# Attention and two expert layers on one core: the first loads on two queues, masks first, and GpSimd's first rounding moved behind two normalisations

## The chip, the cores and the metric

The program runs on one core of one Trainium2 chip, in one launch. The metric is the device time of that core in microseconds (us). The kernel before takes 1297.48 us, the median of three runs that lie between 1297.32 and 1298.49 us.

A core has five engines that run their own instruction lists and wait for one another by semaphores: TensorE (PE in the profile, with its weight loads as PEld), VectorE (DVE), ScalarE (ACT), GpSimd (POOL) and SyncE (SP). DMA transfers are begun by an instruction on one of them; in the kernel before all are begun by SyncE.

## The reference, cut to what matters

```
x  = attention(q, k, v)      # 2 x 8 heads, 768 positions, 64 wide; keys kept:
                             # the first 4 positions (sinks) and a window of 128
h  = x @ w_in                # 1536 x 512 by 512 x 1024
ln = layernorm(h * softmax(h)) * g_ln
y  = ln @ w_out              # 1536 x 1024 by 1024 x 512
P  = exp(y @ w_gate - max), 8 rounds of dividing by row and by column sums
out = sum over 8 experts e:  P[:, e] * (relu(y @ w1[e]) @ w2[e])
```

Everything is float32. For attention the scores of a query tile are taken with a band of keys and the sinks, a mask is added, and the row is exponentiated, divided by its sum and multiplied by the values.

## The kernel before, in words

The attention stage goes over 8 pairs of heads (p = 0 to 7); the two heads of a pair (h = 0, 1) lie in the lower and the upper 64 partitions of `q_sb` and `k_sb`. A pair has six tiles of 128 queries (t = 0 to 5). For each tile PE makes the scores (L659), DVE adds the mask and takes the row maximum (`mask_max`, L1202), ACT exponentiates (L982), and after two tiles, a batch b, DVE takes the inverse sums (L1210, L1214). Then the probabilities are scaled: DVE does one block (L1217), ACT one (L997), and POOL the two blocks of head 1 (`normalise`, L493). PE turns them (L679), ACT and DVE copy them out (L989, L1223), PE multiplies by the values (L705) and by the sinks' values (L711), and ACT and DVE write the result in two parts into `xw` (L1001, L1233). The work of one pair overlaps with the next: in PE's order `scores(p + 1, 0)` stands between tile 5 of pair p and `pv(p, 0)`, and `turn_sinks(p)` and `turn(p, 2)` stand inside pair p + 1.

All orders are written out by hand, one list for each engine. Four places matter here.

SyncE begins the loads of q and k of pairs 0 and 1 (`load_qk`, four DMAs for each head, 16 in all), waits until the constants are made, then begins the v loads of pair 0, the first segments of `w_in` and `w_out` (256 KB each, into `w_raw`), the small tables `g_col` and `wg_raw`, and the v loads of pair 1. After that, for p from 1 on, it waits until GpSimd has finished with segment p - 1 (`in_done`, `out_done`) and begins segment p; the q and k loads of pair 2 stand behind segment 1 in the list, and so on.

GpSimd fills four constants (L458 to L461), makes `ident` (L463), and then the three masks (L465 to L485). After that it rounds the first segments of the weights (`round_segments(0)`: L500 and L503, each of which waits for its DMA), and goes round the pairs: normalise batch 0, rest of `w_in` (L509), normalise batch 1, rest of `w_out` (L515), normalise batch 2, rounding of the next segments.

PE waits for all five constants and for all eight q and k loads of pair 0 before its first scores. `turn(p, 0)` needs GpSimd's `normalise(p, 0)`, and `scores(1, 0)` the eight loads of pair 1.

At the end of pair 0 ACT copies the gate weights (L1025), for which it waits for `small_loaded`, and DVE, before `mask_max` of pair 1, waits for that copy and subtracts (L1262).

The stages behind attention (h = x @ w_in, the layer norm, y, the gate, 8 experts in 4 units each) are one stream of matmuls on PE.

Of the kernel before, what the change touches and what calls it, by code (L numbers as in the profile page):

```python
# [24 lines left out]
F32 = mybir.dt.float32  # L25
F32R = mybir.dt.float32r
BF16 = mybir.dt.bfloat16
ALU = mybir.AluOpType
# [32 lines left out]
def solu_moe(nc: bass.Bass, n_sink, window, qT, kT, v, w_in, w_out, g_ln, w_gate, w_exp, out):  # L61
# [5 lines left out]
    with ExitStack() as ctx:  # L67
# [143 lines left out]


        qk_loaded = [sem(f"qk_loaded{h}") for h in range(2)]
        v_loaded = [sem(f"v_loaded{h}") for h in range(2)]
# [150 lines left out]


        @block.sync
        def _(sp):
# [18 lines left out]
            def load_segments(j):  # L387

                sp.dma_start(w_raw[:, 0:BANK], w_in[j]).then_inc(win_loaded, 16)
                sp.dma_start(w_raw[:, BANK:2 * BANK], w_out[j]).then_inc(wout_loaded, 16)  # L390

            for h in range(2):
                load_qk(0, h)
            for h in range(2):
                load_qk(1, h)
            sp.wait_ge(consts, 4)
            for h in range(2):
                load_v(0, h)
            load_segments(0)
# [56 lines left out]
        def _(pool):  # L456

            pool.memset(ident[:, :], 0.0).then_inc(consts, 1)  # L458
            pool.memset(ones[:, :], 1.0).then_inc(consts, 1)
            pool.memset(v_sink[:, :], 0.0).then_inc(consts, 1)  # L460
            pool.memset(wg[:, :, :].bitcast(F32), 0.0).then_inc(consts, 1)  # L461
            pool.wait_ge(consts, 4)
            pool.affine_select(out=ident[:, :], in_=ident[:, :], compare_op=ALU.not_equal, fill=1.0,  # L463
                               base=0, pattern=[[-1, P]], channel_multiplier=1).then_inc(consts, 1)
            pool.memset(mask0[:, :], 0.0)  # L465
            pool.memset(mask1[:, :], 0.0)
            pool.memset(mask2[:, :], 0.0).then_inc(masks, 1)
            pool.wait_ge(masks, 1)

# [14 lines left out]
            pool.memset(mask0[:, 0:NS], 0.0)  # L484
            pool.memset(mask1[:, 0:NS], 0.0).then_inc(masks, 1)  # L485

            def normalise(p, b):
# [29 lines left out]

            round_segments(0)
            for p in range(PAIRS):
                normalise(p, 0)  # L520
                rest_w_in(p)
                normalise(p, 1)
                rest_w_out(p)
                normalise(p, 2)
                if p + 1 < PAIRS:
                    round_segments(p + 1)
# [120 lines left out]
        def _(pe):  # L647
            def scores(p, t):

                if t == 0:  # L650
                    pe.wait_ge(qk_loaded[p % 2], 128 * (p // 2 + 1))
                for h in range(2):
                    k = 2 * t + h
                    n = STEPS * p + k
                    if n >= S_BANKS:
                        pe.wait_ge(scores_read, n - S_BANKS + 1)
                    rows_h = slice(64 * h, 64 * h + 64)
                    w, at = width(t), k_from(t, h)
                    pe.matmul(bank(k % S_BANKS)[:, 0:w], q_sb[rows_h, p % 2, t * P:(t + 1) * P],  # L659
                              k_sb[rows_h, p % 2, k_at(t), at:at + w], start=True, stop=True).then_inc(scores_full, 1)  # L660
# [76 lines left out]
            def h1_half(T, n):  # L737
# [15 lines left out]
                if n == 1:  # L753
                    last.then_inc(h1_full, 1)

            pe.wait_ge(consts, 5)
            scores(0, 0)
            for p in range(PAIRS):
# [218 lines left out]
        @block.scalar  # L977
        def _(act):
            def exp_tile(p, k):
                act.wait_ge(scores_read, STEPS * p + (k + 1))  # L980
# [35 lines left out]
            for p in range(PAIRS):  # L1016
# [6 lines left out]
                if p == 0:  # L1023
                    act.wait_ge(small_loaded, 32)
                    act.activation(wg[:, :, WG_AT:WG_AT + EXPERTS], wg_raw[:, :, :], ACT.Copy).then_inc(wg_ready, 1)  # L1025

# [496 lines left out]
```

## Time and profile before

| | |
|---|---|
| median of three runs | 1297.48 us (1297.32 to 1298.49) |
| the profiled execution | 1299.42 us, its span 1297.6 us |
| PE busy | 1254.1 us (97%) |
| PE weight loads | 1099.6 us (85%) |
| DVE / ACT / POOL busy | 593.6 / 442.1 / 709.5 us |
| mean granted clock of TensorE | 0.996 of full speed |

The span runs from the first to the last instruction. Attention takes the first 110 us of it, some 12.6 us for a pair from pair 2 on; from there to the end PE is busy nearly without a break. The profile gives the granted clock of TensorE as a share of full speed, where 1.00 is 2.4 GHz and 0.50 is 1.2 GHz. "SPq" rows are DMAs being begun by SyncE: the time in them is that of the issue, not of the transfer.

### The profile page before, as it was taken

To read this page: it belongs to the slowest core of one execution; us is meant where nothing else is said; L and a number is where in the kernel's file an instruction comes from. 1 tells how busy PE (TensorE), PEld (TensorE's weight loads), DVE (VectorE), ACT (ScalarE), POOL (GpSimd) and SP (SyncE) were. 2 spreads that over 40 slices of the span, in tenths; PEclk is the share of its full clock that TensorE was granted. 3 is DMA by queue.
4 is the path that set the end of the run, shared out by engine and by line. 5 is a ranking of instruction groups with operands and counts; after the bars stand their busy time and mean duration, and the time that the engine had idled before them with its cause. 6 is when DMAs were issued, how large, how long until landed. Compare 5 with 4: busy or idle time off the path is not lost.

```text
span 1297.6 us, 18947 instructions
## 1 busy us (share of the span) xinstructions
PE 1254.1 (97%) x6462; PEld 1099.6 (85%) x6462; DVE 593.6 (46%) x1155; ACT 442.1 (34%) x1015; POOL 709.5 (55%) x768
## 2 busy tenths in 40 slices
PE   6889999999999999999999999999999999999998
PEld 3556899998888888888888888888888888888887
DVE  4885645334554444444444444444444444444444
ACT  4774534332225222222222222222222222223222
POOL 4553313575555555555555555555555555555652
PEclk8999999999999999999999999999999999999999
DMA  6651000001111111111111111111111111111102
GB/s 156 162 146 46 1 1 1 17 34 33 33 33 33 33 33 33 33 32 32 32 32 32 32 33 32 34 35 35 38 36 33 32 32 32 32 32 33 34 17 97
DMA packets 62607, 53.17 MB, mean 41 GB/s; under 512 B 9824, under 2 KB 49760, under 8 KB 62560
## 3 DMA queue, kind: packets, MB, share of 16 engines
q1 hardware_dynamic: 62560, 52.57, 14.0%
q8 instruction: 27, 0.44, 0.1%
q14 instruction: 20, 0.16, 0.0%
HBM read 49.40 MB, written 3.15 MB: 40 GB/s over the span
## 4 chain that ended last, share of the span: by engine, by line
PE 71%; POOL 14%; issue 10%; DVE 2%; ACT 1%; SPq 1%; POOLq 0%; DMA 0%; DVEq 0%
PE ps L733 23%; PE ps L735 22%; PE ps L734 22%; POOL ring L612 6%; POOL ring L604 5%; POOL ring L600 2%; PE ps L705 1%; PE ps L679 1%; PE ps L783 1%; PE ps L659 1%; DVE pT L1223 1%; PE ps L711 1%; POOL probs L493 1%; ACT probs L982 1%; PE ps L920 1%
## 5 line engine op out<-in xcount | busy, mean ns | idle before, releaser
L612 POOL TENSOR_TENSOR ring<-sums,ring 128x384 fp32r<-128x384 f32 x192 | 194.9, 1016 | 413.7 <-ACT sums L1144 413.7
L1456 DVE SCALAR_TENSOR_TENSOR acc<-ps,gate_now,acc 128x512 f32<-128x512 f32 x336 | 252.3, 751 | 224.8 <-PE ps L735 224.8
L733 PE MATMUL ps<-ring 128*128 128x512 f32 x768 | 303.5, 395 | 17.2 <-POOL ring L612 13.9
L734 PE MATMUL ps<-ring 128*128 128x512 f32 x768 | 299.6, 390 | 0.0
L735 PE MATMUL ps<-ring 128*128 128x512 f32 x768 | 299.4, 390 | 0.0
L1129 ACT ACTIVATE sums<-ps 128x384 f32<-128x384 f32 x192 | 94.4, 492 | 541.2 <-PE ps L735 541.2
L1432 DVE TENSOR_TENSOR sums<-ps,sums 128x384 f32<-128x384 f32 x192 | 106.8, 556 | 259.2 <-ACT sums L1129 162.3
L733 PEld LDWEIGHTS ps<-ring 128*128 128x128 f32 x768 | 144.1, 188 | 54.7 <-issue 27.2
L735 PEld LDWEIGHTS ps<-ring 128*128 128x128 f32 x768 | 144.2, 188 | 30.8
L734 PEld LDWEIGHTS ps<-ring 128*128 128x128 f32 x768 | 144.2, 188 | 25.9
L733 PE MATMUL ps<-xw,ring 128*128 128x384 f32 x448 | 152.4, 340 | 0.5 <-ACT sums L1129 0.4
L735 PE MATMUL ps<-xw,ring 128*128 128x384 f32 x448 | 151.0, 337 | 0.0
L734 PE MATMUL ps<-xw,ring 128*128 128x384 f32 x448 | 150.9, 337 | 0.0
L733 PE MATMUL ps<-xw,w_b 128*128 128x384 f32 x448 | 150.5, 336 | 0.0
L735 PE MATMUL ps<-xw,w_b 128*128 128x384 f32 x448 | 150.3, 336 | 0.0
L734 PE MATMUL ps<-xw,w_b 128*128 128x384 f32 x448 | 150.0, 335 | 0.0
L1143 ACT ACTIVATE ring<-sums 128x384 fp32r<-128x384 f32 x192 | 100.4, 523 | 118.5 <-DVE sums L1432 118.4
L1144 ACT ACTIVATE sums<-sums 128x384 f32<-128x384 f32 x192 | 98.1, 511 | 0.0
L733 PEld LDWEIGHTS ps<-xw,ring 128*128 128x128 f32 x448 | 84.1, 188 | 2.9 <-ACT sums L1129 0.7
L734 PEld LDWEIGHTS ps<-xw,w_b 128*128 128x128 f32 x448 | 84.3, 188 | 2.0
L733 PEld LDWEIGHTS ps<-xw,w_b 128*128 128x128 f32 x448 | 84.1, 188 | 1.8
L734 PEld LDWEIGHTS ps<-xw,ring 128*128 128x128 f32 x448 | 84.1, 188 | 1.8
(141 smaller groups left out, 1728.1 us busy)
## 6 DMA issues: line engine op xcount, KB each, us to landing
w_in<-w_exp SPq DMA_DIRECT2D x64, 256.0 KB, 3.3
w_raw<-w_exp SPq DMA_DIRECT2D x64, 128.0 KB, 2.7
w_raw<-w_exp SPq DMA_DIRECT2D x32, 256.0 KB, 3.1
q_sb<-qT SPq DMA_DIRECT2D x16, 192.0 KB, 3.8
k_sb<-kT SPq DMA_DIRECT2D x16, 192.0 KB, 3.9
v_sb<-v SPq DMA_DIRECT2D x16, 192.0 KB
out<-acc SPq DMA_DIRECT2D x12, 256.0 KB, 2.0
k_sb<-kT SPq DMA_DIRECT2D x16, 128.0 KB, 3.6
```

The costliest lines, as they stand in the source:

```text
L493: last = pool.tensor_tensor(a, a, a_stat[:, A_INV, k:k + 1].to_broadcast([P, width(t)]), ALU.mult)
L600: pool.tensor_scalar(w2c(0, 0, 2 * BANK), w2_raw(0, 2 * BANK), 1.0, 0.0, ALU.mult, ALU.add).then_inc(w2_hi, 1)
L604: last = pool.tensor_tensor(w2c(1, i * BANK, BANK), w2_raw(i * BANK, BANK), w2c(0, i * BANK, BANK).bitcast(F32), ALU.subtract)
L612: pool.tensor_tensor(h_at(1, i, b * BLK, BLK), c_sum(m), h_at(0, i, b * BLK, BLK).bitcast(F32), ALU.subtract).then_inc(h_lo_pool, 1)
L733: pe.matmul(o, ws[0], xs[0], start=first, stop=False, skip_group_check=True)
L734: pe.matmul(o, ws[0], xs[1], start=False, stop=False, skip_group_check=True)
L735: return pe.matmul(o, ws[1], xs[0], start=False, stop=last, skip_group_check=True)
L1129: act.activation(part_sum(m, s), a_bank(s), ACT.Copy).then_inc(part_copied, 1)
L1143: act.activation(h_at(0, i, b * BLK, BLK), c_sum(m), ACT.Relu)
L1144: act.activation(c_sum(m), c_sum(m), ACT.Relu).then_inc(h_hi_out, 1)
L1432: dve.tensor_tensor(c_sum(m), at, part_sum(part, s), ALU.add).then_inc(c_summed, 1)
L1456: dve.scalar_tensor_tensor(out=acc[:, T, :], in0=y_bank(u, T), scalar=gate_now[:, T:T + 1], in1=acc[:, T, :], op0=ALU.mult, op1=ALU.add).t ...
```

## The change

The first pair's q and k loads are begun by two engines, SyncE for head 0 and ScalarE for head 1, with six DMAs each in place of four: the first 256 columns of q and k come first and count on a semaphore of their own, `qk_first`. PE starts its first scores when these have landed, without waiting for the constants; tile 1 waits for the constants, tile 2 for the rest of the pair's loads. SyncE's list goes on with the v loads of pair 0 (for which it waits on two constants, no longer four), and only then with q and k of pair 1. GpSimd makes the masks first and the last three constants behind them. In pair 0 it normalises batches 0 and 1 before it rounds the first segments of the weights. ScalarE waits for the five constants before it copies the gate weights.

```diff
+        def load_first_qk(queue, h):
+            rows_h = slice(64 * h, 64 * h + 64)
+            q_h, k_h = qT[0, h][0:DH], kT[0, h][0:DH]
+            n, at = 2 * P, h * NS
+            queue.dma_start(q_sb[rows_h, 0, 0:n], q_h[:, 0:n]).then_inc(qk_first, 16)
+            queue.dma_start(k_sb[rows_h, 0, 0, at:at + n], k_h[:, 0:n]).then_inc(qk_first, 16)
+            queue.dma_start(k_sb[rows_h, 0, QT // 2:QT - 1, at:at + n],
+                            k_h[:, P:SEQ - P].rearrange("d (a n) -> d a n", n=n)).then_inc(qk_loaded[0], 16)
+            queue.dma_start(q_sb[rows_h, 0, n:SEQ], q_h[:, n:SEQ]).then_inc(qk_loaded[0], 16)
+            queue.dma_start(k_sb[rows_h, 0, 1:QT // 2, at:at + n],
+                            k_h[:, n:SEQ].rearrange("d (a n) -> d a n", n=n)).then_inc(qk_loaded[0], 16)
+            at = (1 - h) * n
+            queue.dma_start(k_sb[rows_h, 0, :, at:at + NS],
+                            k_h[:, 0:NS].unsqueeze(1).to_broadcast([DH, QT - 1, NS])).then_inc(qk_loaded[0], 16)
...
+            load_first_qk(sp, 0)
+            sp.wait_ge(consts, 2)
             for h in range(2):
-                load_qk(0, h)
+                load_v(0, h)
             for h in range(2):
                 load_qk(1, h)
-            sp.wait_ge(consts, 4)
-            for h in range(2):
-                load_v(0, h)
             load_segments(0)
...
-            pool.memset(ident[:, :], 0.0).then_inc(consts, 1)
-            pool.memset(ones[:, :], 1.0).then_inc(consts, 1)
-            pool.memset(v_sink[:, :], 0.0).then_inc(consts, 1)
-            pool.memset(wg[:, :, :].bitcast(F32), 0.0).then_inc(consts, 1)
-            pool.wait_ge(consts, 4)
-            pool.affine_select(out=ident[:, :], ...).then_inc(consts, 1)
             pool.memset(mask0[:, :], 0.0)
             pool.memset(mask1[:, :], 0.0)
             pool.memset(mask2[:, :], 0.0).then_inc(masks, 1)
+            pool.memset(ident[:, :], 0.0).then_inc(consts, 1)
+            pool.memset(v_sink[:, :], 0.0).then_inc(consts, 1)
...
+            pool.wait_ge(consts, 2)
+            pool.affine_select(out=ident[:, :], ...).then_inc(consts, 1)
+            pool.memset(ones[:, :], 1.0).then_inc(consts, 1)
+            pool.memset(wg[:, :, :].bitcast(F32), 0.0).then_inc(consts, 1)
...
-            round_segments(0)
             for p in range(PAIRS):
                 normalise(p, 0)
-                rest_w_in(p)
+                if p > 0:
+                    rest_w_in(p)
                 normalise(p, 1)
+                if p == 0:
+                    round_segments(0)
+                    rest_w_in(0)
                 rest_w_out(p)
...
-                if t == 0:
+                if t == 0 and p == 0:
+                    pe.wait_ge(qk_first, 64)
+                if (p, t) == (0, 2) or p > 0 and t == 0:
                     pe.wait_ge(qk_loaded[p % 2], 128 * (p // 2 + 1))
...
-            pe.wait_ge(consts, 5)
             scores(0, 0)
+            pe.wait_ge(consts, 5)
...
         def _(act):
+            load_first_qk(act, 1)
...
                     act.wait_ge(small_loaded, 32)
+                    act.wait_ge(consts, 5)
```

Where the instructions now stand is shown in three places. First GpSimd, behind the masks and up to the end of pair 0's batch 1, before:

```order
22 L485 MEMSET mask1 128x4
23 L500 TENSOR_SCALAR xw<-w_raw 128x512 [waits win_loaded]
24 L503 TENSOR_SCALAR w_end<-w_raw 128x512 [waits wout_loaded]
25 L493 TENSOR_TENSOR probs<-probs,a_stat 128x128 [waits norm_link]
26 L493 TENSOR_TENSOR probs<-probs,a_stat 128x256
27 L509 TENSOR_TENSOR xw<-w_raw,xw 128x512 [waits in_hi]
28 L493 TENSOR_TENSOR probs<-probs,a_stat 128x260 [waits norm_link]
29 L493 TENSOR_TENSOR probs<-probs,a_stat 128x260
30 L515 TENSOR_TENSOR w_end<-w_raw,w_end 128x512 [waits out_hi]
```

and GpSimd at the same place with the change:

```order
22 L501 MEMSET wg 128x896
23 L509 TENSOR_TENSOR probs<-probs,a_stat 128x128 [waits norm_link]
24 L509 TENSOR_TENSOR probs<-probs,a_stat 128x256
25 L509 TENSOR_TENSOR probs<-probs,a_stat 128x260 [waits norm_link]
26 L509 TENSOR_TENSOR probs<-probs,a_stat 128x260
27 L516 TENSOR_SCALAR xw<-w_raw 128x512 [waits win_loaded]
28 L519 TENSOR_SCALAR w_end<-w_raw 128x512 [waits wout_loaded]
29 L525 TENSOR_TENSOR xw<-w_raw,xw 128x512 [waits in_hi]
30 L531 TENSOR_TENSOR w_end<-w_raw,w_end 128x512 [waits out_hi]
```

The four scalings of probabilities stand ahead of everything that waits for `w_raw`.

Second SyncE, from its last load for pair 0 to the first segment of the weights, before (the rows from 9 on are pair 1's):

```order
8 L379 DMA k_sb<-kT 64x5x4
9 L372 DMA q_sb<-qT 64x768
16 L379 DMA k_sb<-kT 64x5x4
17 L383 DMA v_sb<-v 128x384 [waits consts]
20 L384 DMA v_sink<-v 4x64
21 L389 DMA w_raw<-w_in 128x512
24 L401 DMA wg_raw<-w_gate 128x32
```

and with the change, where rows 7 to 10 are v of pair 0 and rows 11 to 18 are q and k of pair 1:

```order
1 L373 DMA q_sb<-qT 64x256
6 L381 DMA k_sb<-kT 64x5x4
7 L400 DMA v_sb<-v 128x384 [waits consts]
10 L401 DMA v_sink<-v 4x64
11 L389 DMA q_sb<-qT 64x768
18 L396 DMA k_sb<-kT 64x5x4
19 L406 DMA w_raw<-w_in 128x512
22 L417 DMA wg_raw<-w_gate 128x32
```

The last load of pair 1 moves from place 16 to place 18 of the list, the first segment of `w_in` from 21 to 19.

Third PE, its first scores, before:

```order
1 L659 MATMUL ps<-k_sb,q_sb 128x128 [waits qk_loaded0,consts]
2 L659 MATMUL ps<-k_sb,q_sb 128x128
3 L659 MATMUL ps<-k_sb,q_sb 128x256 x2
4 L659 MATMUL ps<-k_sb,q_sb 128x260 [waits scores_read] x8
5 L679 MATMUL ps<-ident,probs 128x128 [waits probs_scaled,probs_ready0]
```

and with the change:

```order
1 L680 MATMUL ps<-k_sb,q_sb 128x128 [waits qk_first]
2 L680 MATMUL ps<-k_sb,q_sb 128x128
3 L680 MATMUL ps<-k_sb,q_sb 128x256 [waits consts]
4 L680 MATMUL ps<-k_sb,q_sb 128x256
5 L680 MATMUL ps<-k_sb,q_sb 128x260 [waits scores_read,qk_loaded0]
6 L680 MATMUL ps<-k_sb,q_sb 128x260 [waits scores_read] x7
7 L700 MATMUL ps<-ident,probs 128x128 [waits probs_scaled,probs_ready0]
```

One wait at the start has become three, one before each of the first three tiles.

## Rows read from the trace of the kernel before

**Rows 1.** Timeline of PE: start us, us, engine line op, operands [idle before].
```profile
8.69 6.09 PE L659 MATMUL ps<-k_sb,q_sb 64*128 64x128 f32 x24 [8.69 <-DMA k_sb<-kT]
14.71 0.55 PE L679 MATMUL ps<-ident,probs 128*128 128x128 f32 x3
18.35 0.90 PE L679 MATMUL ps<-ident,probs 128*128 128x128 f32 x3 [3.09 <-POOL probs L493]
19.18 0.80 PE L659 MATMUL ps<-k_sb,q_sb 64*128 64x128 f32 x4
...
22.58 1.97 PE L679 MATMUL ps<-ident,probs 128*128 128x128 f32 x8
...
33.56 0.49 PE L659 MATMUL ps<-k_sb,q_sb 64*128 64x128 f32 x4
34.59 0.87 PE L705 MATMUL ps<-pT,v_sb 128*64 128x256 f32 x8 [0.54 <-DVE pT L1223]
35.39 0.70 PE L659 MATMUL ps<-k_sb,q_sb 64*128 64x256 f32 x4
36.02 1.09 PE L679 MATMUL ps<-ident,probs 128*128 128x128 f32 x8
...
46.12 0.49 PE L659 MATMUL ps<-k_sb,q_sb 64*128 64x128 f32 x4
```
**Rows 2.** Timeline of POOL, same columns.
```profile
5.69 0.10 POOL L485 MEMSET mask<- 128x4 f32 x1
...
16.74 0.62 POOL L503 TENSOR_SCALAR w_end<-w_raw 128x512 fp32r<-128x512 f32 x1 [0.46 <-DMA w_raw<-w_out]
17.32 0.97 POOL L493 TENSOR_TENSOR probs<-probs,a_stat 128x128 f32<-128x128 f32 x2
...
20.63 1.27 POOL L515 TENSOR_TENSOR w_end<-w_raw,w_end 128x512 fp32r<-128x512 f32 x1
22.75 1.25 POOL L493 TENSOR_TENSOR probs<-probs,a_stat 128x260 f32<-128x260 f32 x2 [0.84 <-DVE a_stat L1214]
```
**Rows 3.** Timeline of DVE, same columns.
```profile
12.32 0.18 DVE L1214 RECIPROCAL a_stat<-a_stat 128x4 f32<-128x4 f32 x1
...
24.59 0.69 DVE L1223 COPY pT<-ps 128x512 f32<-128x512 f32 x1 [1.07 <-PE ps L679]
```
**Rows 4.** Timeline of SyncE's DMA issues: start us, us, line, what.
```profile
0.72 0.58 SPq L372 DMA_DIRECT2D q_sb<-qT  x1
...
5.24 0.61 SPq L379 DMA_DIRECT2D k_sb<-kT  x1
...
10.44 0.61 SPq L379 DMA_DIRECT2D k_sb<-kT  x1
...
12.94 0.33 SPq L389 DMA_DIRECT2D w_raw<-w_in  x1
...
14.26 0.43 SPq L401 DMA_DIRECT2D wg_raw<-w_gate  x1
...
27.27 0.61 SPq L379 DMA_DIRECT2D k_sb<-kT  x1
```
**Rows 5.** DMA issues at 10.44, 14.26 and 27.27: KB, us to landing.
```profile
k_sb<-kT SPq DMA_DIRECT2D x1, 5.0 KB, 3.3
...
wg_raw<-w_gate SPq DMA_DIRECT2D x1, 16.0 KB, 2.8
...
k_sb<-kT SPq DMA_DIRECT2D x1, 5.0 KB, 4.3
```
**Rows 6.** Windows: stretch, length, busy us (count) PE, PEld, DVE, ACT, POOL; clock; DMA; GB/s.
```profile
5.00:8.60 3.60, 0.00 (x0) 0.00 (x0) 0.00 (x0) 0.00 (x0) 0.73 (x4) 1.00 0.95 217
14.64:18.05 3.41, 0.62 (x4) 0.31 (x3) 0.53 (x2) 1.56 (x6) 1.93 (x4) 1.00 0.78 245
21.46:24.88 3.42, 3.42 (x15) 2.44 (x16) 2.27 (x9) 1.88 (x6) 1.94 (x4) 0.50 0.54 164
106.80:110.20 3.40, 2.44 (x14) 1.17 (x14) 2.71 (x7) 2.56 (x7) 2.49 (x3) 1.00 0.02 5
110.20:113.60 3.40, 3.40 (x13) 2.43 (x11) 1.56 (x7) 1.11 (x5) 1.25 (x2) 0.50 0.53 154
```

More of the change, by code:

```diff
@@ L210, in bank @@
             return ps[:, b * BANK:(b + n) * BANK]
+        qk_first = sem("qk_first")
         qk_loaded = [sem(f"qk_loaded{h}") for h in range(2)]
@@ L456, in _ @@
         def _(pool):
-            pool.memset(ident[:, :], 0.0).then_inc(consts, 1)
-            pool.memset(ones[:, :], 1.0).then_inc(consts, 1)
-            pool.memset(v_sink[:, :], 0.0).then_inc(consts, 1)
-            pool.memset(wg[:, :, :].bitcast(F32), 0.0).then_inc(consts, 1)
-            pool.wait_ge(consts, 4)
-            pool.affine_select(out=ident[:, :], in_=ident[:, :], compare_op=ALU.not_equal, fill=1.0,
-                               base=0, pattern=[[-1, P]], channel_multiplier=1).then_inc(consts, 1)
             pool.memset(mask0[:, :], 0.0)
@@ L485, in _ @@
             pool.memset(mask1[:, 0:NS], 0.0).then_inc(masks, 1)
+            pool.wait_ge(consts, 2)
+            pool.affine_select(out=ident[:, :], in_=ident[:, :], compare_op=ALU.not_equal, fill=1.0,
+                               base=0, pattern=[[-1, P]], channel_multiplier=1).then_inc(consts, 1)
+            pool.memset(ones[:, :], 1.0).then_inc(consts, 1)
+            pool.memset(wg[:, :, :].bitcast(F32), 0.0).then_inc(consts, 1)
             def normalise(p, b):
@@ L754, in h1_half @@
                     last.then_inc(h1_full, 1)
+            scores(0, 0)
             pe.wait_ge(consts, 5)
-            scores(0, 0)
             for p in range(PAIRS):
```

## The prediction, made before the changed kernel had run

> **What bounds the kernel now.** The page comes first: PE is busy 97% of the span, and behind attention it hardly pauses, so a change in the first 20 us is worth what it moves the start of that stream and nothing more. The next view is the timeline of the first 40 us, PE's first. PE begins at 8.69, when the last load for pair 0 has landed. It runs through the scores of all six tiles and the first half of `turn(0, 0)`, and then stands idle for 3.09 us until 18.35, waiting for GpSimd's scaled probabilities [rows 1]. GpSimd's own timeline says why: the inverse sums were ready at 12.50 [rows 3], but GpSimd stood at `round_segments(0)`, whose second DMA let it go at 16.74; the scaling ran only at 17.32 [rows 2]. So two things set the start: the landing of q and k, and a wait for a weight segment that the probabilities don't need. The windows show a third: TensorE's clock goes to half (1.2 GHz) behind the stretch from 14.64 to 18.05, in which PE was busy 0.62 us of 3.41, and is still at half up to 24.88 [rows 6]. The price of that is in the rows too: eight transposes take 1.97 us at half clock and 1.09 us at full [rows 1].
>
> From pair 2 on the rows repeat with a period of 12.56 us (`scores(2, 0)` at 33.56, `scores(3, 0)` at 46.12 [rows 1]). DVE's copy at 24.59 [rows 3] is the first instruction that already lies on this pattern; so the gain is what that copy moves, unless something behind it is late.
>
> **The change, part by part.**
>
> Loads of pair 0. Before, SyncE begins 8 DMAs from 0.72 on, one each 0.65 us (8 from 5.24 to 10.44 give the same), and the last, begun at 5.24, lands 3.3 us later [rows 4, 5] (the load begun at 5.24 took as long as the one at 10.44). Now each of two queues has 6: the last begins at 0.72 + 5 x 0.65 = 3.97 and lands at about 7.3. The bytes say nearly the same: about 1034 KB at the 217 GB/s that the DMA engines moved when they were 0.95 busy [rows 6] take 4.8 us, from 2.1 on, so 6.9. I take 7.3 for tile 2. The first two tiles come earlier: their loads land at about 4.5, the masks end at about 4.5 (5.79 less the constants that stood ahead, plus two memsets [rows 2]), the fifth constant at about 5.8. This part has no price and no gain of its own, since tile 2 follows at 7.3 in any case. Tile 2 began at about 10.3 before (the eight matmuls of the first two tiles come ahead of it), so pair 0's scores move 3.0 us earlier, and `turn(0, 0)` from 14.71 to about 11.7. What ScalarE's six issues cost no row of before shows, for it begins no DMA there. Bounds: no less than SyncE's 0.33 each, and at most the 0.65 of SyncE's pace counted twice over. By 0.65 ScalarE is free at 4.6, with one table load left to do before its first exponential, whose maximum comes at about 5.8; that costs nothing. At 1.3 each, head 1's last load would begin at 7.2 and land at 10.5, and tile 2 would be as late as before.
>
> GpSimd. The inverse sums of batch 0 come at 12.50 - 3.0 = 9.5, the scaling takes 0.97 and ends at 10.5, before PE wants it at 12.2. The 3.09 us of idle time are gone whole: `turn(0, 0)` ends at about 12.8 instead of 19.18.
>
> What is late next: `scores(1, 0)`, which comes at once, waits for pair 1's loads. These have moved back in SyncE's list, behind the v loads. Six DMAs to 4.6, the v loads 1.85 us (from 10.44 + 0.65 to 12.94), eight times 0.65: the last begins at 0.72 + 3.9 + 1.85 + 7 x 0.65 = 11.0 and lands 3.3 later, at 14.3 [rows 4, 5]. The DMA engines allow about that: 1034 + 386 + 1034 KB at 200 to 217 GB/s from 2.1 on end at 13.4 to 14.4. Ends: 13.9 if the pace is a little quicker, 15.5 if two queues in parallel slow each other. I take 14.5, and 14.6 for `scores(1, 0)`. Before it was 19.18: a gain of 4.6 us here. So of the 6.4 us by which `turn(0, 0)` is early, 1.8 are lost to this new wait.
>
> The Trainium skill (Trainium Kernel Development and Optimization, Key Constraints) says that DMAs issued from several engines run on the same 16 DMA engines, and that this saves the issue time alone. The share of 0.95 at 217 GB/s agrees; by the rule the second queue buys the 1.3 us of two issues out of sixteen for pair 1 and no bandwidth, which is the sum that I made from the issue rows.
>
> From `scores(1, 0)` to DVE's copy before took 24.59 - 19.18 = 5.41 us, at half clock. At full clock the same PE work takes about 3.0 us: 0.49 for the scores, 0.80 for eight matmuls with v, 0.63 and 1.07 for the next scores and the transposes (by the starts from 34.59 on [rows 1]). But DVE isn't there before 17.9: it waits for the gate table, begun at 14.26 - 1.3 = 13.0 and landed at 15.8 [rows 4, 5], then does 2.1 us of its own work (subtraction, two masks, normalisation). So the copy moves by 24.59 - 20.0 = 4.6 at half clock, and by 24.59 - 17.9 = 6.7 at full.
>
> Which clock? PE is idle from 12.8 to 14.6. A stretch with 2.44 us busy of 3.40 was enough of a pause for half clock afterwards [rows 6], and here it is some 1.8 us of pause, so half clock around pair 1's start is more likely than not. [...]
>
> Behind the copy the next bound is SyncE again. Pair 2's loads stand behind segment 1, which waits for GpSimd's L515, ended at 21.90 [rows 2]. Now GpSimd waits for the `w_out` segment only after batch 1: that lands 0.6 to 1.3 us earlier than 16.7 (SyncE is 1.3 earlier at that place), then 0.62 + 1.27 + 1.27 us: 18.6 to 19.3, so 2.6 to 3.3 earlier. The last load of pair 2, landed at 27.27 + 4.3 = 31.6 before [rows 4, 5], comes at 28.3 to 29.0. `scores(2, 0)` stood at 33.56 and PE idled 0.54 behind it [rows 1], so up to 34.1 would have done: a cap on the gain of 34.1 - 29.0 = 5.1 to 5.8 us. GpSimd's other work in pair 1 has room: batch 2 of pair 0 starts at about 19 instead of 22.75, and batch 0 of pair 1 is wanted by PE some 5 us after it was done.
>
> Later stages. The granted clock also falls to half at 110.20, for 3.40 us, at the change from attention to the next stage [rows 6]; at half clock PE's stream loses 1.7 us there. Whether that stretch comes again depends on where the pauses fall; I count 0, with 1.7 either way for the range. Nothing else is changed.
>
> Sum: between 4.6 (half clock) and the cap of 5.1 to 5.8 I take 5.0. The profiled execution had 1299.42 us and a span of 1297.6; it would become 1294.4 with a span of 1292.6. The median of the runs was 1.9 under it, so the forecast is 1297.48 - 5.0 = 1292.5 us.
>
> **Rivals.**
>
> A, landing later and a slower clock: two queues with small rows slow each other, pair 1 lands at 15.5 to 16.5, and the half clock lasts into pair 1. For it: the engines are already 0.95 busy. Against: a longer list was always served at SyncE's pace. Gain 19.1 - 16 = about 3, less 0.8 of transposes at half clock: 1295.3.
>
> B, full clock through pair 1, or the fall at 110.20 gone: the gain is at the cap, 5.8, or 5.0 + 1.7 = 6.7: 1291. For it: PE's pause is shorter than before. Against: the 2.44 us row.
>
> C, the change does nothing because ScalarE's issues are slow: at 1.3 us or more each pair 0 lands as late as before, and yet the wait for `w_raw` is gone. `turn(0, 0)` ends at 15.8, `scores(1, 0)` comes at 15.9: gain 3.2. At 1.7 us each it would be about 1.9: 1295.6.
>
> D, slower: the clock. If the pause before `scores(1, 0)` puts TensorE at half, and the sparse work of pair 1 doesn't bring it back as it did by 24.88 but only a whole pair later, PE's matmuls on the loop pay twice: about 6.2 us of the 12.56 at full clock, so + 6.2 us: 1297.48 - 5.0 + 6.2 = 1298.7, and 1304.9 with two such pairs. It decides as soon as half clock lasts more than 5 us of PE work beyond that of before. Against: at half clock PE had 3.42 of 3.42 us to do and was back at full at once.
>
> **How the numbers follow.** Forecast case 0.57, A 0.15, B 0.15, C 0.08, D 0.05. The forecast's own range is 1291.6 to 1293.6. With A, B and C taken in up to the last tenth on each side it is 1290.4 to 1295.2. About 0.2% (2.6 us) is what a measurement can tell from no change, so faster means under 1294.9: the forecast case, B and not quite half of A and C give 0.83. Slower by over 0.2% is D with two pairs, 0.03, since D with one pair is still within the bound; within 0.2% has 0.14.
>
> **What would show it.** Right: PE's first scores at about 4.5 to 5, tile 2 at about 7.3; no wait for GpSimd inside `turn(0, 0)`; instead a wait of 1 to 3 us for `k_sb` before `scores(1, 0)` at about 14.6; GpSimd's wait for `w_raw` behind four scalings; DVE's copy of pair 0's batch 1 at 19 to 20; the period of 12.56 us from there. Wrong: pair 1's loads landed past 16, ScalarE's issues of over 1 us, a clock at half past 25 us, or pair 2's loads holding PE near 28.5.

## The result

The changed kernel takes 1293.76 us, the median of 12 runs (1293.29 to 1295.53), against 1297.55 us of the kernel before (12 runs on the same chips, 1296.70 to 1298.99). The ratio is 0.9974 with a 95% interval of 0.9966 to 0.9981: faster by 3.8 us by the medians and by 3.4 by the ratio, between 2.5 and 4.4. Forecast were 1292.5 us and a gain of 5.0.

The profiled execution took 1293.96 us with a span of 1292.2 us; before they were 1299.42 and 1297.6. The two spans differ by 5.4 us, more than the medians, and the traces say where. In both, attention ends in its steady pattern, and the same eight matmuls of pair 7 stand at 110.01 before and at 106.15 after: 3.86 us. Before, half clock set in just there. The timeline of the kernel before (start us, us, engine, line, operands), PE's row and then DVE's next maximum:

```profile
110.01 1.39 PE L705 MATMUL ps<-pT,v_sb 128*64 128x256 f32 x8 [0.96 <-DVE pT L1223]
...
119.07 1.22 DVE L1278 TENSOR_REDUCE stat<-ps 128x1 f32<-128x1024 f32 x1 [2.06 <-PE ps L735]
```

and the same two places of the changed kernel:

```profile
106.15 0.87 PE L726 MATMUL ps<-pT,v_sb 128*64 128x256 f32 x8 [0.96 <-DVE pT L1247]
...
113.67 1.23 DVE L1302 TENSOR_REDUCE stat<-ps 128x1 f32<-128x1024 f32 x1 [2.06 <-PE ps L756]
```

The distance grows from 3.86 to 5.40 us in that stretch, which is the stretch at half clock [rows 6], and stays so to the end. The prediction allowed 1.7 us for it either way; here it costs 1.54. The profiled execution of the kernel before has it (mean granted clock 0.996, where most of its other runs have 0.997), and so have the traces of five of the twelve kernels below, where the clock falls between 104.7 and 109.6 us; it is not shown to belong to the change. What is left between the two traces is the 3.86 us, and the medians differ by 3.8.

### The profile page after: what moved, and what is told of

Read it like the earlier page. It is cut to its first block, busy times and chain, and to the rows that moved or that the text cites. A ratio compares the mean times of both kernels' runs of the same rounds, so it can differ in the third digit from the quotient of the medians.

```text
span 1292.2 us, 18952 instructions
## 1 busy us (share of the span) xinstructions
PE 1251.2 (97%) x6462; PEld 1096.7 (85%) x6462; DVE 595.6 (46%) x1155; ACT 441.7 (34%) x1015; POOL 709.2 (55%) x768
## 4 chain that ended last, share of the span: by engine, by line
PE 71%; POOL 14%; issue 10%; DVE 2%; ACT 1%; SPq 1%; POOLq 0%; DMA 0%; DVEq 0%
PE ps L754 23%; PE ps L756 22%; PE ps L755 22%; POOL ring L631 6%; POOL ring L623 5%; POOL ring L619 2%; PE ps L726 1%; PE ps L700 1%; PE ps L804 1%; DVE pT L1247 1%; PE ps L732 1%; ACT probs L1005 1%; PE ps L680 1%; PE ps L941 1%; POOL probs L509 0%
```

## The profile after

Line numbers are those of the changed kernel: scores L680, transposes L700, matmuls with v L726, GpSimd's scaling L509, rounding L516 and L519, rests L525 and L531, the gate table L1049 on ACT and L1286 on DVE. PE's timeline, which answers to [rows 1]:

```profile
4.73 1.94 PE L680 MATMUL ps<-k_sb,q_sb 64*128 64x128 f32 x8 [4.73 <-DMA k_sb<-kT]
8.60 4.34 PE L680 MATMUL ps<-k_sb,q_sb 64*128 64x260 f32 x16 [1.93 <-DMA k_sb<-kT]
12.86 0.87 PE L700 MATMUL ps<-ident,probs 128*128 128x128 f32 x6
15.44 0.56 PE L680 MATMUL ps<-k_sb,q_sb 64*128 64x128 f32 x4 [1.70 <-DMA k_sb<-kT]
...
18.56 1.36 PE L700 MATMUL ps<-ident,probs 128*128 128x128 f32 x8
...
21.56 0.87 PE L726 MATMUL ps<-pT,v_sb 128*64 128x128 f32 x8 [1.00 <-DVE pT L1247]
...
29.70 0.49 PE L680 MATMUL ps<-k_sb,q_sb 64*128 64x128 f32 x4
...
42.27 0.49 PE L680 MATMUL ps<-k_sb,q_sb 64*128 64x128 f32 x4
```

`turn(0, 0)` is one piece of six transposes now; the 3.09 us for GpSimd are gone, and a wait of 1.70 us for pair 1's loads stands in their place. But there is a second new wait, 1.00 us for DVE's copy ahead of 21.56. Pair 2 comes at 29.70 instead of 33.56, and pair 3 12.57 us after it.

GpSimd's timeline, which answers to [rows 2], has the scalings first:

```profile
11.18 1.06 POOL L509 TENSOR_TENSOR probs<-probs,a_stat 128x128 f32<-128x128 f32 x2 [5.80 <-DVE a_stat L1238]
13.47 1.25 POOL L509 TENSOR_TENSOR probs<-probs,a_stat 128x260 f32<-128x260 f32 x2 [1.22 <-DVE a_stat L1238]
15.97 0.62 POOL L516 TENSOR_SCALAR xw<-w_raw 128x512 fp32r<-128x512 f32 x1 [1.26 <-DMA w_raw<-w_in]
...
17.23 1.26 POOL L525 TENSOR_TENSOR xw<-w_raw,xw 128x512 fp32r<-128x512 f32 x1
18.46 1.27 POOL L531 TENSOR_TENSOR w_end<-w_raw,w_end 128x512 fp32r<-128x512 f32 x1
```

ACT's timeline and then DVE's show who holds the copy, the row at 20.74 that answers to 24.59 of [rows 3]:

```profile
16.98 0.23 ACT L1049 ACTIVATE wg<-wg_raw 128x32 fp32r<-128x32 f32 x1 [0.80 <-DMA wg_raw<-w_gate]
```

```profile
17.24 1.30 DVE L1286 TENSOR_TENSOR wg<-wg_raw,wg 128x32 fp32r<-128x32 f32 x1 [1.85 <-ACT wg L1049]
18.47 0.28 DVE L1226 CUSTOM_DVE_ANT_0 probs<-ps,mask 128x128 f32<-128x128 f32 x1
...
18.89 0.87 DVE L1234 TENSOR_SCALAR a_stat<-a_stat 128x4 f32<-128x4 f32 x1
...
20.74 0.68 DVE L1247 COPY pT<-ps 128x512 f32<-128x512 f32 x1
```

The copy has no idle time ahead of it: PE's transposes ended at 19.92 and DVE came to them 0.8 us later. It had stood 1.85 us for the gate table and then worked without a pause from 17.24 on.

The issues of the last loads of pair 0, of pair 1 and of the gate table (start us, us of the issue; ACTq is ScalarE's queue), and the time until each landed:

```profile
3.99 0.62 SPq L381 DMA_DIRECT2D k_sb<-kT  x1
...
4.27 0.63 ACTq L381 DMA_DIRECT2D k_sb<-kT  x1
...
10.93 0.61 SPq L396 DMA_DIRECT2D k_sb<-kT  x1
...
13.17 0.43 SPq L417 DMA_DIRECT2D wg_raw<-w_gate  x1
```

```profile
k_sb<-kT SPq DMA_DIRECT2D x1, 5.0 KB, 4.1
...
k_sb<-kT ACTq DMA_DIRECT2D x1, 5.0 KB, 4.3
...
k_sb<-kT SPq DMA_DIRECT2D x1, 5.0 KB, 4.5
...
wg_raw<-w_gate SPq DMA_DIRECT2D x1, 16.0 KB, 3.8
```

SyncE's were begun where the prediction put them (3.97, 11.0, 13.0), ScalarE's last at 4.27 instead of 3.97; each landed 0.8 to 1.2 us later than [rows 5] let expect. The clock, in three stretches of the windows view:

```profile
14.64:15.74 1.10, 0.30 (x4) 0.30 (x4) 0.76 (x5) 0.76 (x4) 0.07 (x1) 1.00 1.09 345
15.74:19.15 3.41, 3.41 (x19) 1.87 (x16) 1.91 (x6) 1.03 (x5) 3.12 (x4) 0.50 0.27 91
19.16:22.57 3.41, 2.40 (x21) 1.47 (x21) 3.34 (x11) 2.17 (x9) 1.88 (x4) 1.00 0.51 160
```

It was at half (1.2 GHz) behind the pause before `scores(1, 0)`, for 3.4 us where it had been 6.8 before. The clock column has to be read with the matmuls beside it: until the first change that it shows it reads 1.00, whatever the pace. In `loads_only` below it is 1.00 until 109 us, and yet eight transposes at 21.81 take 1.97 us, as they do at half clock in [rows 1]. Seven of the twelve runs of the changed kernel have a mean clock of 1.000; that doesn't say that pair 1 ran at full clock in them.

## The experiments

Twelve kernels were run in three groups of four; every ratio is against the kernel before on the same chip, with its 95% interval. Where rows are quoted, line numbers are of the kernel named. A trace is of one execution, and in seven of the twelve kernels (`loads_only`, `gate_late`, `pool_gate`, `one_queue`, `two_queues_whole`, `warm_before`, `warm_after`) that execution took 1.2 to 3.0 us more than the kernel's median. So such a trace shows what happened in it, and not by itself what made the median.

**First: which part does it?** `pool_only` is the kernel before with GpSimd's order alone; `loads_only` is the full change with GpSimd's old order.

```diff
# pool_only, on the kernel before
-            round_segments(0)
             for p in range(PAIRS):
                 normalise(p, 0)
-                rest_w_in(p)
+                if p > 0:
+                    rest_w_in(p)
                 normalise(p, 1)
+                if p == 0:
+                    round_segments(0)
+                    rest_w_in(0)
```

> The kernel before with GpSimd's new order alone (loads, masks and queues as before). Theory G (GpSimd's wait for w_raw was the cost, and the gate table on DVE is what is late next): turn(0,0) runs through at 14.7 to 15.6, scores(1,0) follow at about 15.8, pair 1's loads landed at 13.7, the gate table lands at 17.1 as before, DVE's copy of pair 0's batch 1 comes at 20.8: about 1293.8 us, the same as the full change within 0.5 us. Rival L (the early loads are a real part of the gain): the copy comes later than 21.5 and the time is 1295 us or more.

> The full change with GpSimd's old order (first segments rounded ahead of the scalings). Theory G: GpSimd is let go by w_out at about 16.5 to 17.3, turn(0,0) ends at about 19 as before, and the time is 1297 to 1297.5 us, no change. Rival L: the loads bring at least 1 us by themselves, 1296.5 us or less.

Measured: `pool_only` 1295.62 us, ratio 0.9987 (0.9978 to 0.9996); `loads_only` 1297.48 us, ratio 0.9997 (0.9987 to 1.0006). GpSimd's order by itself gives about 2 us, the loads by themselves nothing that can be told from zero, both together 3.8. (By its interval the first is worth 0.5 to 2.9 us, the second at most 1.7, so that the two may well add up to the whole.) So theory G holds for `loads_only` and fails on the size of `pool_only`, where the rival's time came out, though its copy (later than 21.5) did not. PE's timeline of `pool_only`:

```profile
14.25 0.88 PE L682 MATMUL ps<-ident,probs 128*128 128x128 f32 x6
15.05 0.49 PE L662 MATMUL ps<-k_sb,q_sb 64*128 64x128 f32 x4
...
21.97 0.87 PE L708 MATMUL ps<-pT,v_sb 128*64 128x128 f32 x8 [1.83 <-DVE pT L1226]
...
24.23 2.16 PE L682 MATMUL ps<-ident,probs 128*128 128x128 f32 x8
...
31.00 0.49 PE L662 MATMUL ps<-k_sb,q_sb 64*128 64x128 f32 x4
```

`scores(1, 0)` came at 15.05, even earlier than in the full change, since pair 1's loads stand ahead of v here. DVE's copy was at 21.15, near the 20.8 that were expected. But behind PE's pause of 1.83 us before 21.97 the clock was at half from 23.3 to 26.8 (2.16 us for eight transposes), and that is most of the rest: pair 2 at 31.00 against 29.70, of which the copy accounts for 0.4.

In `loads_only` PE waited 3.70 us for GpSimd, and its transposes of pair 1 ran at the half pace:

```profile
17.57 0.90 PE L697 MATMUL ps<-ident,probs 128*128 128x128 f32 x3 [3.70 <-POOL probs L509]
...
21.81 1.97 PE L697 MATMUL ps<-ident,probs 128*128 128x128 f32 x8
```

Its copy came at 23.82 and pair 2 at 32.79, 0.8 us earlier than before. So up to pair 2 the traces have 0.77 us for the loads, 2.56 for GpSimd's order and 3.86 for both: the two parts nearly add up, and about 0.9 of what `pool_only` lacks went behind its copy, where its clock was at half.

**Second: is the gate table what is late next?** `gate_late` moves both gate-table steps of the full change from the end of pair 0 to the end of pair 1; `pool_gate` does the same on `pool_only`.

```diff
# gate_late, on the changed kernel, in ScalarE's and in VectorE's list
-                if p == 0:
+                if p == 1:
                     act.wait_ge(small_loaded, 32)
...
-                if p == 0:
+                if p == 1:
                     dve.wait_ge(wg_ready, 1)
```

> The full change with the two gate-table steps (ACT's copy, DVE's subtraction) moved from the end of pair 0 to the end of pair 1. Theory G: DVE no longer stands until 17.2, the 1.30 us subtraction leaves this place, and the copy follows PE's transposes at 19.9 to 20.0 instead of 20.74: 0.7 us faster than the full change, 1293.1 us. Rival S (pair 2's loads behind GpSimd's segment, landed at 29.5, bind already) or rival C (the subtraction costs as much at its new place): 1293.8 us, with PE waiting for k_sb before scores(2,0), or with the period of pair 1 to 2 longer than 12.56.

> The kernel before with GpSimd's new order and the gate-table steps at the end of pair 1. Theory G: scores(1,0) at 15.8, transposes until 20 to 21 by the clock, copy right behind: 1293 to 1294 us. If half clock is on until past 21 the copy comes at 21.2 and the time is 1294.2; if PE's pause has gone, so that full clock stays, the copy comes at about 18.5 to 19 and the time is 1292, unless pair 2's loads (landed at 29.6) hold it at 1293.5.

Measured: `gate_late` 1293.81 us, 0.9972 (0.9961 to 0.9983), the same as the full change; `pool_gate` 1294.48 us, 0.9977 (0.9968 to 0.9987). In `gate_late` DVE's copy came at 18.28, 2.5 us earlier than in the full change, and now it waited 0.99 us for PE, not PE for it: the gate table no longer held it. Not all of the 2.5 us is the gate table's, for in this execution PE also did pair 1 at full clock (eight transposes in 1.09 us). At the pace of the full change they ended at 19.92, so without the gate steps the copy could have come 0.8 us earlier there, as was expected; most of the other 1.6 is the clock's. In the traced execution the gain was taken back, and more, at pair 2's q and k, as rival S has it. The time 1293.81 is rival S's too. PE's timeline of `gate_late`, and DVE's:

```profile
17.15 1.09 PE L700 MATMUL ps<-ident,probs 128*128 128x128 f32 x8
...
30.47 0.80 PE L680 MATMUL ps<-k_sb,q_sb 64*128 64x128 f32 x4 [2.81 <-DMA k_sb<-kT]
```

```profile
18.28 0.69 DVE L1247 COPY pT<-ps 128x512 f32<-128x512 f32 x1 [0.99 <-PE ps L700]
...
30.15 0.19 DVE L1286 TENSOR_TENSOR wg<-wg_raw,wg 128x32 fp32r<-128x32 f32 x1 [0.94 <-ACT wg L1049]
```

The landing at 30.4 is the cap that the prediction worked out from SyncE's list (28.3 to 29.0 there). The last of these loads was begun at 25.19, as in the full change (25.10), but took 5.2 us to land where it took 4.0 there; why is open. In this wait the clock fell to half for 6.8 us, and pair 2 took 14.44 us (to 44.91) instead of 12.57. This execution took 1296.69 us, the longest of seven; how much of it is in the median is not shown. DVE's last row gives the bare price of the subtraction: 0.19 us where GpSimd is idle, against 1.30 in the full change, where GpSimd ran L525. In `pool_gate` the copy came at 19.36, PE waited 2.57 us at the same place, and pair 2 took 14.40 us, again with 6.8 us at half clock.

**Third: with pair 2's loads out of the way.** `gate_late_qk2` begins pair 2's loads before segment 1; `qk2_only` does this on the full change.

```diff
# gate_late_qk2 (on gate_late) and qk2_only (on the changed kernel), SyncE
+            sp.wait_ge(scores_full, STEPS)
+            for h in range(2):
+                load_qk(2, h)
             for p in range(1, PAIRS):
-                if p >= 2:
+                if p >= 3:
                     sp.wait_ge(scores_full, STEPS * (p - 1))
```

> The full change, with the gate-table steps at the end of pair 1 and pair 2's q and k loads ahead of segment 1 in SyncE's list. Theory Q (with the gate table out of the way, the wait of 2.81 us for pair 2's loads before scores(2,0) is all that took the gain back): scores(2,0) follow the transposes at about 27.6 instead of 29.70, the wait is gone, and so is the half clock behind it: 1293.8 - 2.1 = 1291.7 us. Rival P (segment 1, which now lands about 1 us later, holds GpSimd and through it the transposes of pair 1): 1293 us or more, with PE waiting for GpSimd's scaling in pair 1.

> The full change with pair 2's q and k loads ahead of segment 1 in SyncE's list, the gate-table steps left where they are. Theory G (DVE, standing for the gate table, decides the first pair and pair 2's loads are just in time): no change, 1293.8 us within 0.5. Rival S (pair 2's loads are the binding wait of the full change): 1293 us or less.

Measured: `gate_late_qk2` 1294.24 us, 0.9972 (0.9962 to 0.9982), runs from 1292.47 to 1295.71; `qk2_only` 1294.21 us, 0.9971 (0.9959 to 0.9982). The second is as theory G has it, no change: pair 2's loads don't bind while DVE stands for the gate table. The first is a miss on the time (1291.7 were expected). Its one trace, of the fastest run, has pair 2 at 27.33 as expected, and its span is 1290.6 us. But the trace also shows rival C, the price of the gate steps at the new place (PE's timeline, then DVE's):

```profile
27.33 0.49 PE L683 MATMUL ps<-k_sb,q_sb 64*128 64x128 f32 x4
...
41.40 0.49 PE L683 MATMUL ps<-k_sb,q_sb 64*128 64x128 f32 x4 [0.67 <-DMA k_sb<-kT]
```

```profile
29.89 0.19 DVE L1289 TENSOR_TENSOR wg<-wg_raw,wg 128x32 fp32r<-128x32 f32 x1 [0.94 <-ACT wg L1052]
```

DVE now waits 0.94 us there for ACT's copy, which stands behind two exponentials, and its next copy comes 0.7 us later in the pair than in the full change. Another 0.67 us is PE's wait for pair 3's loads ahead of 41.40. So pair 2 takes 14.07 us instead of 12.57; the pair after it takes only 11.98, and at pair 7 1.5 us of the 2.4 are left. Rival P's time (1293 or more) came out, but not its mechanism: the trace has no wait of PE for GpSimd's scaling in pair 1. Six of the nine runs are 1.6 to 3.2 us slower than the traced one; why stays open.

**Fourth: the queue and the split.** `one_queue` lets SyncE begin all twelve loads of pair 0; `two_queues_whole` keeps two queues but the four whole loads of each head, and PE waits for all of them.

```diff
# one_queue, on the changed kernel
             load_first_qk(sp, 0)
+            load_first_qk(sp, 1)
...
-            load_first_qk(act, 1)
# two_queues_whole, on the changed kernel: load_first_qk has the four DMAs of load_qk
-                    pe.wait_ge(qk_first, 64)
-                if (p, t) == (0, 2) or p > 0 and t == 0:
+                    pe.wait_ge(qk_loaded[0], 128)
+                if p > 0 and t == 0:
```

> The full change with all twelve loads of pair 0 begun by SyncE, head 0's six first; ScalarE begins none. Theory I (the second queue's worth is the issue time): the last of pair 0 is begun at 0.72 + 11 x 0.65 = 7.9 and lands at 11.2 instead of 8.5, the last of pair 1 is begun at 14.9 and lands at 18.2 to 18.7, so scores(1,0) at 18.5 instead of 15.44 and the gate table at about 20.5: about 3 us slower than the full change, 1296.8 us. Rival B (the DMA engines are the bound and the issue pace doesn't matter): pair 0 lands at about 8.5 to 9 all the same, and the time is 1294 to 1294.5.

> The full change with pair 0's loads on two queues but whole, four DMAs for each head as before, and PE waiting for all of them before its first scores. Theory B (the DMA engines are the bound of these loads; only the early start of tiles 0 and 1 comes from the split): pair 0 lands at about 7.5 to 8.5, PE starts there and does tiles 0 and 1 after it, turn(0,0) ends at 14 to 14.5; SyncE's list is 1.3 us earlier, but pair 1 lands at 15 or later by the engines: 1293.5 to 1294.5, little change. Theory I (issue pace): pair 0 lands at 6.5, pair 1 at 13.5, the gate table at 15.6: 1292.7 us.

Measured: `one_queue` 1297.35 us, 0.9997 (0.9987 to 1.0006): the whole gain is gone. `two_queues_whole` 1294.49 us, 0.9974 (0.9963 to 0.9984), as the full change. PE's timelines of both, in this order:

```profile
10.87 4.79 PE L681 MATMUL ps<-k_sb,q_sb 64*128 64x260 f32 x16 [1.65 <-DMA k_sb<-kT]
...
18.15 0.49 PE L681 MATMUL ps<-k_sb,q_sb 64*128 64x128 f32 x4 [1.15 <-DMA k_sb<-kT]
```

```profile
7.83 4.30 PE L677 MATMUL ps<-k_sb,q_sb 64*128 64x128 f32 x20 [7.83 <-DMA k_sb<-kT]
...
30.05 0.49 PE L677 MATMUL ps<-k_sb,q_sb 64*128 64x128 f32 x4
```

With one queue the issue pace decides (theory I): tile 2 at 10.87, pair 1 at 18.15. That puts the copy at 23.52, 2.8 us later than in the full change and still 1.1 earlier than before; in the traced execution the clock was at half from 23.5 to 30.4, and pair 2 came only at 34.56. With two queues it is the landing that decides pair 0, as theory B has it: eight whole loads had landed by 7.8, where the issue pace with 3.3 us to landing would have given 6.5. Pair 1, though, landed at 14.0 (begun at 9.58, 4.4 us), nearer to theory I's 13.5 than to theory B's 15. Beginning the first two tiles early brought nothing that the time shows. The order of the masks was not run by itself; here PE starts at 7.83, when the masks would have been there in the old order too (5.79), and the time is that of the full change. Pair 2 came 0.35 us later than in the full change.

**Fifth: the clock.** Unread bf16 matmuls 128x256 on a constant tile keep PE busy in its pauses; nothing that is computed changes.

```diff
# warm_before, warm_after, warm_gate_qk2
+            def keep_busy(n):
+                for _ in range(n):
+                    pe.matmul(ps[:, 6 * BANK:6 * BANK + 2 * P], idle_in[:, 0:P], idle_in[:, :], start=True, stop=True,
+                              skip_group_check=True)
# warm_before: keep_busy(34) before scores(0, 0), keep_busy(24) between the halves of turn(0, 0)
# warm_after: keep_busy(16) before scores(0, 0), 8 between tiles 1 and 2, 12 before scores(1, 0)
# warm_gate_qk2: 16, 8 and 10 at the same places of gate_late_qk2
# warm_gate_vlast: as warm_gate_qk2, load_qk(1, h) ahead of load_v(0, h)
```

> The kernel before with matmuls that nobody reads: 34 of bf16 128x256 before PE's first scores and 24 between the two halves of turn(0,0), so that PE is busy while it would wait. Nothing that is computed changes. Theory H (half clock from 18 to 25 cost about 2.5 us of PE work before pair 1's steady pattern): full clock holds from before 18 on, the work from scores(1,0) to DVE's copy takes 3 to 3.5 us instead of 5.4, the copy comes at 22.5, and scores(2,0) at 31.6 to 32, held by pair 2's loads: 1295.6 us. Rival N (the clock was no part of the cost): within 0.5 us of the kernel before.

> The full change with 16 unread matmuls before the first scores, 8 between tiles 1 and 2 and 12 before scores(1,0). Theory G (DVE, standing for the gate table, decides the first pair, at half and at full clock): DVE's copy stays at 20.5 to 20.8; the time is 1293.3 to 1293.8 us, only the slower of the runs (those at 1295) come down. Rival H (the clock is what kept the full change from more): the copy comes at 19.5 or earlier and the time is 1292.7 us or less.

> The full change with gate-table steps at the end of pair 1, pair 2's loads ahead of segment 1, and 16, 8 and 10 unread matmuls in PE's pauses. Theory H (the runs of the same kernel without them lie between 1292.5 and 1295.7 by when the clock first rises, before pair 1 or in it): scores(2,0) at 27.3 or earlier in all runs, median 1292.0 to 1292.6 us with a small spread. Rival N: the median stays at 1294.2.

> As warm_gate_qk2, with pair 1's q and k loads ahead of pair 0's v loads in SyncE's list. Theory V (at full clock and without the gate table, pair 1's landing at 15 is the binding wait): scores(1,0) come at 14 instead of 15, but v lands at about 15.3 and pv(0,0) waits for it, so that 0.3 to 0.5 us are won: 1291.8 us. Rival W (v is wanted as soon as q and k): no gain or 0.3 us lost.

Measured: `warm_before` 1297.31 us, 0.9996 (0.9987 to 1.0005); `warm_after` 1294.68 us, 0.9976 (0.9967 to 0.9985); `warm_gate_qk2` 1293.59 us, 0.9968 (0.9957 to 0.9978); `warm_gate_vlast` 1293.33 us, 0.9968 (0.9956 to 0.9981).

`warm_before` is inconclusive: it didn't do what it was made for. The 24 matmuls ended 1.7 us before GpSimd let PE go, and half clock came all the same, later and for a shorter time:

```profile
18.75 0.55 PE L688 MATMUL ps<-ident,probs 128*128 128x128 f32 x3 [1.70 <-POOL probs L495]
...
21.94 1.97 PE L688 MATMUL ps<-ident,probs 128*128 128x128 f32 x8
...
32.92 0.49 PE L666 MATMUL ps<-k_sb,q_sb 64*128 64x128 f32 x4
```

`warm_after` is a mixed result. Full clock held through pair 0 and pair 1, and the trace shows both of the bounds behind it, DVE's copy and then pair 2's loads (PE's timeline, then DVE's):

```profile
17.47 0.71 PE L687 MATMUL ps<-k_sb,q_sb 64*128 64x260 f32 x4
19.97 0.87 PE L733 MATMUL ps<-pT,v_sb 128*64 128x128 f32 x8 [1.79 <-DVE pT L1260]
...
29.39 0.80 PE L687 MATMUL ps<-k_sb,q_sb 64*128 64x128 f32 x4 [1.22 <-DMA k_sb<-kT]
```

```profile
16.52 0.20 DVE L1300 TENSOR_TENSOR wg<-wg_raw,wg 128x32 fp32r<-128x32 f32 x1 [2.04 <-ACT wg L1062]
...
19.14 0.68 DVE L1260 COPY pT<-ps 128x512 f32<-128x512 f32 x1
```

DVE's copy came at 19.14, 1.6 us earlier than in the full change: here it is rival H's copy (19.5 or earlier) that came out, and not theory G's (20.5 to 20.8). It was not PE's clock that moved it, for PE still waited 1.79 us for DVE. The gate table had landed 0.7 us earlier, and the subtraction took 0.20 us where it had taken 1.30. But pair 2 comes at 29.39 against 29.70, held by its loads, and then the clock was at half for 6.8 us from 29.0 on: pair 3 comes at 43.95, 1.7 us later than in the full change. The median of `warm_after` is no better than that of the full change, as theory G had it; that the slower runs would come down was wrong, they are still there (1295.95, the traced one). So this kernel says nothing on what full clock throughout would be worth.

The last two kernels are the lowest of all, but their intervals overlap with that of the full change (0.9966 to 0.9981): whether either beats it is not shown. `warm_gate_qk2` was expected at 1292.0 to 1292.6 with a small spread by theory H and at 1294.2 by rival N; 1293.59 with runs from 1292.53 to 1295.95 is neither. In it pair 2 came at 27.42 and pair 3 at 40.95, 13.5 us later, again with the gate steps in that pair. In `warm_gate_vlast` `scores(1, 0)` came at 15.21 and not at 14, since tile 2 came only at 9.18 and the clock was at half from 9.4 to 12.8; PE reached these scores without a wait, so that theory V had nothing to show. Pair 2 came at 27.95.

## Why the prediction was right, and where it was off

The forecast was 1292.5 us in a range of 1290.4 to 1295.2, and faster; measured were 1293.76. Direction and main mechanism hold: GpSimd's wait for `w_raw` was the cost, `turn(0, 0)` runs through, and pair 1's loads are a new wait. The gain is 3.8 where 5.0 were forecast, and it lies just outside the forecast's own range (up to 1293.6). By its steps:

- GpSimd's order: right. The inverse sums were forecast for 9.5 and came at about 11.1, mostly because tile 2 was late, and `turn(0, 0)` ended at 13.7 instead of 12.8.
- Loads of pair 0, tile 2 at 7.3: off by 1.3 us (8.60). This is the first term that was mis-sized. Of it 0.3 us is ScalarE's last issue, begun at 4.27 instead of 3.97, and the rest the way from issue to landing: it was taken as 3.3 us from the row at 10.44 and was 4.1 on SyncE's queue and 4.3 on ScalarE's. [rows 5] had 4.3 us as well, for the load at 27.27. The sum from bytes (6.9) was too short as well. This is rival A's mechanism, with a smaller price than A gave it.
- ScalarE's issues: 0.60 to 0.86 us each, free at 4.93; the table load ended at 6.2, so that its first exponential began 0.2 us behind the maximum, long before tile 2 at 8.60. Rival C is out.
- `scores(1, 0)` at 14.6: came at 15.44, by the same 1.2 us on the way to landing (4.5 instead of 3.3).
- From there to DVE's copy: this step named the wrong engine. The prediction took PE's half-clock work, 14.6 + 5.4 = 20.0, and put DVE's readiness at 17.9. DVE came at 20.74. Of the 2.8 us between, 1.2 are the gate table's landing (16.98 instead of 15.8), 0.3 are ACT's copy of it, which the sum left out, and 1.4 are DVE's own work, which took 3.5 us instead of 2.1: the subtraction took 1.30 us where it had taken 0.48 before, and the 128x4 instruction behind it 0.87 instead of 0.16. `warm_after` bears it out: there the gate table was 0.7 us earlier and the subtraction took 0.20 us, and the copy came at 19.14. That the step came within 0.8 us of the forecast all the same is luck: PE's transposes, which the prediction had as the bound, ended at 19.92, close by the engine that was the bound.
- The clock: in the profiled execution half for 3.4 us at pair 1's start, as the more likely case had it; the sum for that case was 4.6, and 5.0 was taken. But it decided less than was argued. PE's transposes ended at 19.92, before DVE was free.
- The cap by pair 2's loads: right in kind, and seen as a wait of 2.81 us in `gate_late`, 2.57 in `pool_gate` and 1.22 in `warm_after`. It was put at a gain of 5.1 to 5.8, with a landing at 28.3 to 29.0. The landing was 29.1 in the full change (25.10 and 4.0), 29.4 in `warm_after` and 30.4 in `gate_late`: by 33.56 + 0.54 less these the cap is 5.0, 4.7 and 3.7, and the full change with its 3.86 is below its own.
- The stretch at half clock at 110 us: present in the profiled run of before, absent in that of after. Three of the twelve runs of the changed kernel stand at 1295.05 to 1295.53; whether they are those with such a stretch is not shown.

Rival B (full clock through pair 1, 5.8 us) stays open in its size: `warm_after` had the full clock there, and pair 2's loads held it at 29.39, a gain of 4.2 at `scores(2, 0)`; in that wait its clock fell, and the gain was lost again. Rival D did not come about in the full change. Its mechanism did, one pair later, in `gate_late`, `pool_gate` and `warm_after`: half clock for 6.8 us in pair 2, which then took 1.8 to 2.0 us more and not 6.2.

## What to carry to other kernels

When a wait is taken out, follow every engine to the next join, not only the one that waited: here the engine that had stood idle (DVE) became the one that was late, for a 16 KB table that PE first reads at 270 us. A list of loads on one queue has to be costed by place and by landing: a second queue took 6 issues out of one list of 12, while the way to landing was 1 us longer than assumed. With all 12 on one queue (`one_queue`) the gain was gone; with the old list of 8 on one queue (`pool_only`) 2 us of it were there; with 4 on each of two (`two_queues_whole`) it was whole. The split into more loads cost issue time and brought nothing that the runs show; what it cost, the second queue paid for.

## What the runs showed of the hardware

- A small DVE instruction that starts while a GpSimd instruction is running can be held until that one ends. In the full change the 128x32 subtraction began at 17.24, 0.01 us behind GpSimd's L525, and ended at 18.54, 0.05 behind its end; the 128x4 instruction at 18.89 took 0.87 us and ended 0.03 behind the end of L531. Before, the subtraction began 0.4 us ahead of such an end and took 0.48. With GpSimd idle it took 0.19 (`gate_late`), and 0.20 in `warm_after`, where it and GpSimd's instruction began together at 16.52. Not every instruction is held: mask and maximum (L1226), which reads the scores in `ps`, took 0.28 us beside L531 as elsewhere. The Trainium skill (GPSIMD Engine Reference, Architecture) says that GpSimd's read and write ports to SBUF are shared with VectorE; the rows agree in kind, and no row separates a port from another cause.
- The way from issue to landing of a 5 KB load is not one number. It was 3.3 us at 10.44 and 4.3 at 27.27 before [rows 5], both with one queue, 2.9 and 3.3 in `one_queue` (issues at 7.92 and 14.86), 4.1 to 4.3 with two queues, 4.5 for pair 1's last, when ScalarE had long stopped beginning loads, and 5.2 once in `gate_late`. So the second queue alone doesn't explain the longer way.
- Pauses of PE of 1.7 to 1.8 us were followed by half clock in the full change, in `pool_only`, `one_queue`, `two_queues_whole` and `warm_before`, in the pause itself or up to 2.1 us behind it; a pause of 1.79 us in `warm_after` and one of 1.36 in `gate_late` were not. Half clock lasted 3.4 or 6.8 us each time. Before the column's first change the pace can be half while the column reads 1.00 (1.97 us for eight transposes in `loads_only`).
